# Products of zeros on TensorE in the waits of the first two units

## The reference

```python
for t in range(S):
    state = alpha[:, :, t, :, None] * state + np.einsum('bhd,bhe->bhde', k[:, :, t], v[:, :, t])
    y[:, :, t] = np.einsum('bhd,bhde->bhe', q[:, :, t], state)
```

## Time and profile before

| what | value |
|---|---|
| median of 3 runs | 1319.24 us |
| profiled execution | 1318.9 us |
| its span, first to last instruction | 1317.0 us |
| TensorE busy | 1300.2 us |
| mean granted TensorE clock | 0.997 |
| VectorE, ScalarE, GpSimd busy | 841.1, 607.8, 536.4 us |

### The profile page before, as it was taken

How to read it: one execution, slowest core, us unless ns; L and a number is a source line. 1 busy time by engine, 2 the same in 40 slices (tenths; PEclk the granted TensorE clock), 3 DMA queues, 4 the chain that set the end, 5 groups by cost and what they waited for, 6 DMA issues and landing times.

```text
span 1317.0 us, 26258 instructions
## 1 busy us (share of the span) xinstructions
PE 1300.2 (99%) x10472; PEld 1072.7 (81%) x10472; DVE 841.1 (64%) x1129; ACT 607.8 (46%) x1051; POOL 536.4 (41%) x454
## 2 busy tenths in 40 slices
PE   6999999999999999999999999999999999999999
PEld 6878888888888888888888888888888888888887
DVE  7787767665676765576766567676657645654455
ACT  3666343366434347533336743434753433653332
POOL 1671948611755831453861175583145311100011
PEclk9899999999999999999999999999999999999999
DMA  5535353255245236335335434423633332533330
GB/s 199 179 120 174 93 199 90 85 172 172 86 145 156 75 102 200 114 108 201 89 100 161 169 97 144 145 85 94 215 106 106 96 100 84 152 96 104 99 92 31
DMA packets 84028, 165.77 MB, mean 126 GB/s; under 512 B 30146, under 2 KB 31683, under 8 KB 83908
## 3 DMA queue, kind: packets, MB, share of 16 engines
q1 hardware_dynamic: 83616, 163.97, 39.9%
q10 hardware_dynamic: 292, 0.13, 0.0%
HBM read 157.99 MB, written 6.08 MB: 125 GB/s over the span
## 4 chain that ended last, share of the span: by engine, by line
PE 94%; DVE 3%; issue 1%; ACT 1%; DMA 0%; ACTq 0%; DVEq 0%
PE ps_o L578 15%; PE ps_h L578 14%; PE ps_h L579 14%; PE ps_h L580 14%; PE ps_o L579 14%; PE ps_o L580 14%; PE ps_att L450 2%; PE ps_att L547 1%; DVE w_lo L756 1%; PE ps_att L523 1%; PE ps_att L551 1%; PE ps_att L556 1%; PE ps_att L505 1%; DVE elu_out L769 1%; DVE g_lo L773 0%
## 5 line engine op out<-in xcount | busy, mean ns | idle before, releaser
L756 DVE TENSOR_TENSOR w_lo<-w_stage,w_hi 128x768 fp32r<-128x768 f32 x288 | 332.9, 1156 | 28.8 <-ACT w_hi L960 25.1
L578 PE MATMUL ps_o<-g_hi,w_lo 128*128 128x512 f32 x864 | 342.4, 396 | 0.3 <-DVE g_lo L773 0.3
L578 PE MATMUL ps_h<-x_hi,w_lo 128*128 128x512 f32 x858 | 335.1, 391 | 1.9 <-DVE x_lo L763 1.3
L579 PE MATMUL ps_o<-g_lo,w_hi 128*128 128x512 f32 x864 | 336.7, 390 | 0.0
L580 PE MATMUL ps_o<-g_hi,w_hi 128*128 128x512 f32 x864 | 336.6, 390 | 0.0
L579 PE MATMUL ps_h<-x_lo,w_hi 128*128 128x512 f32 x858 | 334.0, 389 | 0.0
L580 PE MATMUL ps_h<-x_hi,w_hi 128*128 128x512 f32 x858 | 333.9, 389 | 0.0
L991 ACT ACTIVATE g_hi<-ps_h 128x512 fp32r<-128x512 f32 x184 | 110.0, 598 | 473.9 <-PE ps_h L580 473.9
L777 DVE SCALAR_TENSOR_TENSOR g_lo<-ps_h,g_hi 128x512 fp32r<-128x512 f32 x184 | 126.9, 690 | 249.7 <-ACT g_hi L991 249.4
L960 ACT CAST w_hi<-w_stage 128x768 fp32r<-128x768 f32 x288 | 239.4, 832 | 13.9 <-DMA w_stage<-in_w 12.9
L285 POOL TENSOR_TENSOR products<-blocks 128x384 f32<-128x384 f32 x150 | 196.2, 1322 | 81.9 <-DVE scores L692 76.3
(11 more groups left out here) (111 smaller groups left out, 1025.5 us busy)
## 6 DMA issues: line engine op xcount, KB each, us to landing
w_stage<-in_w SPq DMA_DIRECT2D x288, 384.0 KB, 3.1
k_level<-in_k SPq DMA_DIRECT2D x12, 512.0 KB, 5.5
q_low<-in_q SPq DMA_DIRECT2D x12, 512.0 KB, 6.5
alpha<-in_a SPq DMA_DIRECT2D x12, 512.0 KB, 4.1
v_tok<-in_v SPq DMA_DIRECT2D x12, 512.0 KB, 4.7
p_rows<-p_norm SPq DMA_DIRECT2D x6, 1024.0 KB, 9.1
out<-acc SPq DMA_DIRECT2D x18, 256.0 KB, 4.3
blocks<-in_q_blocks SPq DMA_DIRECT2D x10, 384.0 KB, 4.0
```

The source lines that it names most:

```text
L578: nc.tensor.matmul(dst, lhs[1], rhs[0], start=first, stop=False)
L579: nc.tensor.matmul(dst, lhs[0], rhs[1], start=False, stop=False)
L756: nc.vector.tensor_tensor(wl[n % WRING][:], stage[n % STAGE][:], wh[n % WRING][:].bitcast(F32), ALU.subtract).then_inc(w_low, 1)
```

## The change

A helper `zeros(bank, count)` issues `count` products of a 128x128 stationary and a 128x128 moving operand, both the first 128 columns of the cleared buffer `SC[0]`. They write zeros into 128 columns of a bank that the next operation overwrites, and signal no semaphore. They are issued between two groups of waits, as follows: four ahead of the pairs (1, 4), two ahead of (1, 5), two ahead of (1, 6), four ahead of `transpose_k(0)`, three ahead of `outer(0)`: fifteen in all. In `early_pairs` the waits for `e_in`, `e_q` and `e_k` move behind those for `e_mask`, `e_rect` and `st_ready`, and behind the products of zeros; in `transpose_k` the two early waits change places. TensorE waits once for `sc_clear` behind the first state.

```diff
--- before.py
+++ after.py
@@ -105,6 +105,9 @@
 for lag in range(LEVELS - 2):
     EARLY_ORDER += [(0, lag + 2), (1, lag)]
 EARLY_ORDER += [(1, LEVELS - 2), (1, LEVELS - 1)]
+
+
+FILLED = {(1, LEVELS - 3): 4, (1, LEVELS - 2): 2, (1, LEVELS - 1): 2}
 
 
 
@@ -460,12 +463,12 @@
                     pe.wait_ge(k_up, lev(u, l - 1))
                 level(level_banks(u, l), u % 2, l).then_inc(step_done, 1)
 
+            def zeros(bank, count):
+
+                for i in range(count):
+                    nc.tensor.matmul(bank[:, 0:P], SC[0][:, 0:P], SC[0][:, 0:P], start=True, stop=True)
+
             def early_pairs(u, l):
-                if l == 0:
-                    pe.wait_ge(e_in[u], 32)
-                else:
-                    pe.wait_ge(e_q[u], l)
-                    pe.wait_ge(e_k[u], l)
                 if 2 <= l < MASKED + 2:
                     pe.wait_ge(e_mask[u], l - 1)
                 elif l >= MASKED + 2:
@@ -473,6 +476,12 @@
                 if u == 1 and l == 1:
                     pe.wait_ge(st_ready, 1)
                 banks = ps_l[l % 2][u]
+                zeros(banks[0], FILLED.get((u, l), 0))
+                if l == 0:
+                    pe.wait_ge(e_in[u], 32)
+                else:
+                    pe.wait_ge(e_q[u], l)
+                    pe.wait_ge(e_k[u], l)
                 if l == LEVELS - 1:
                     level(banks, u, l).then_inc(e_step[u], 1)
                     return
@@ -495,8 +504,9 @@
 
             def transpose_k(g):
                 if g < EARLY:
+                    pe.wait_ge(e_rect[g // 2], LEVELS - 1 - MASKED)
+                    zeros(kt_bank(g), 4 if g == 0 else 0)
                     pe.wait_ge(e_k[g // 2], LEVELS)
-                    pe.wait_ge(e_rect[g // 2], LEVELS - 1 - MASKED)
                 else:
                     pe.wait_ge(k_up, lev(g // 2, LEVELS - 1))
                     bank_free(g // 2, BANK_AT["K", 0] + g % 2)
@@ -509,6 +519,7 @@
             def outer(u):
                 if u < LEAD:
                     pe.wait_ge(e_rect[u], LEVELS - MASKED)
+                    zeros(kv_bank(u), 3 if u == 0 else 0)
                 else:
                     bank_free(u, BANK_AT["KV", 0])
                 o, s = kv_bank(u), u % 2
@@ -619,6 +630,7 @@
                 last.then_inc(o_step, 1)
 
             first_state()
+            pe.wait_ge(sc_clear, 1)
             for u, l in EARLY_ORDER[:-2]:
                 early_pairs(u, l)
             pe.wait_ge(eye_in, 16)
```

## The result

The changed kernel took 1325.66 us in the median of five executions (1322.26 to 1326.57), the kernel before 1319.08 beside it (1318.95 to 1319.44). The ratio is 1.0044, with a 95% interval of 1.0033 to 1.0055. I had forecast 1318.6, with 1317.6 to 1320.6 as the range, and a chance of 0.05 to anything above 1321.9.

What follows compares the result with a forecast made beforehand. TensorE was taken as the bound, its first main product moving the end. Saving 3.0 us of cold work and giving 2.2 back, with late start and VectorE, left minus 0.6: 1318.6 us from 1319.24, range 1317.6 to 1320.6.

Steps and rivals of the forecast that it cites:

- The first steps: From (1, 4) towards `attend(0)`: clock held at 1.00, products of zeros 0.26 us each, pairs (1, 5) ending 37.0 instead of 37.56.
- steps 7 and 8: `attend(0)` takes 1.55 instead of 2.06 us, transposes 2 and 3 start 0.57 earlier; that lead lasts to the first main product.
- that 0.57: Transposes 2 and 3 start 0.57 us earlier, at 41.65; kept, it puts the first main product at 49.7 instead of 50.28.
- the sign that the prediction named for an error in step 7: Transposes 2 and 3 starting directly behind `attend(0)`, instead of waiting for VectorE's late update until 41.65 us.
- The floor I derived from ScalarE: `outer(1)` needs `k_tokens(3)`, ending at about 44.0 us, so it ends at best at 44.45 instead of 45.67: gain at most 1.2.
- The premise that the clock is up from 31 us and falls at 34.2: TensorE in the kernel before: full speed from about 31 to 34.2 us, then half clock for 6.8 us until 41.0.
- the clock falls all the same: Clock at 0.50 when the transposes start at 34.3 us, `attend(0)` ending 2.0 us later, total 1321.2 us; chance 0.12.

Runs made afterwards that it cites:

- e7: Changed kernel, with unit 2's queries and the loads queued behind them waiting for all four `attend` of units 0 and 1 instead of two: 1323.86 us.
- e2_wide: Changed kernel with products of zeros of 256 moving columns instead of 128, half as many (2, 1, 1, 2, 2): 1319.88 us.
- e4_bare: Changed kernel without any products of zeros, only the reordered waits and the one for `sc_clear`: 1319.29 us.
- e3: Changed kernel with the same fifteen products shrunk to 32 weight columns and 16 moving ones: 1324.65 us.
- e5: Changed kernel with eleven tiny products (32 weight columns, 16 moving; counts 4, 2, 2, 3, 0) instead of fifteen full ones: 1321.65 us.
- e8: Kernel before the change, with unit 2's queries and the loads behind them waiting for all four `attend` of units 0 and 1: 1321.12 us.
- e1: The changed kernel run again without any edit: 1324.26 us.
- e6: Changed kernel with thirteen tiny products (32 weight columns, 16 moving; counts 4, 2, 2, 4, 1) instead of fifteen full ones: 1323.65 us.
- e9: Changed kernel with nineteen tiny products (32 weight columns, 16 moving; counts 4, 2, 2, 4, 7) instead of fifteen full ones: 1324.10 us.
- e10: Changed kernel with eleven of its fifteen full products (4, 2, 2, 3, 0): 1321.87 us.

## Why the prediction was wrong

The first steps held. Against the forecast (in brackets) the trace has a filler every 0.25 us (0.26), the transposes at 34.40 (34.3), the pairs (1, 5) at 35.81 to 36.95 (35.85 to 37.0), and a clock of 1.00 throughout. The pairs (1, 4) started at 32.34 us (32.2), so ScalarE slid by 0.4 us, not 0.2, which put `outer(0)` at 38.12 (37.85) and `attend(0)` at 40.20 (39.9):

```profile
33.54 1.06 ACT L941 COPY blocks<-ps_att 16x128 f32<-16x128 f32 x4 [1.07 <-PE ps_o L495]
...
43.36 1.08 ACT L957 COPY k_tok<-ps_o 128x512 f32<-128x512 f32 x2
```

Those are terms that were a little off. What failed is steps 7 and 8, "the rest runs at full clock in both kernels and keeps that 0.57". `attend(0)` took 2.09 us instead of 1.55, with 0.48 from start to start at border 1985; `outer(1)` 1.30 instead of 0.88, with 0.41 at border 2241; and the last `attend` took a silence of 1.95 at border 2497. Transposes 2 and 3 started at 42.29, directly behind `attend(0)`, which is the sign that the prediction named for an error in step 7. The forecast's 49.7 for the first dense product and the measured 52.76 differ by 3.06 us: about 0.65 had been lost by `outer(1)`, 0.3 of it ScalarE's slide; 0.42 were lost in `outer(1)`, and 2.0 from its end to that product. I priced an added instruction by its time on the array and forgot that it also takes a place in the instruction stream. No rival had it, and the bound of the range rested on the engines' waits alone. The signs stood in the trace of before: two silences ended by "issue" at 16 and 20 us, which the prediction passes over, and the instruction queue in the page's DMA section.

The floor I derived from ScalarE (1.2 us of gain) was not the tightest either. From border 2241 to the first record behind 2497 it took 5.3 to 6.5 us wherever TensorE arrived early, and 3.7 us without the loads (e7); from 1985 to 2241 it took 4.0 and 5.0 us in the two traces of the changed kernel. `outer` and `attend` need 3.4 us for 256 instructions at full clock (45.75 to 49.11). So between 41 and 51 us TensorE, once at full speed, runs ahead of its instructions. That is one likely reason why a held clock brought nothing: e2_wide, at full clock from 32.2 us, has its first dense product at 51.41 us, e4_bare, whose clock rises only at 41.8, at 51.34. The same traces show a second reason, the fillers' own place. Those ahead of (1, 4) held its pairs in e2_wide back to 32.87 us, and ScalarE's chain behind them started at 34.07, against 33.14 before the change (and 33.99 in e4_bare, whose pairs ran at half clock). `outer(1)` then began at 45.28 in e2_wide and at 45.57 in e4_bare, so the held clock was worth 0.3 us there; border 2241 then took 0.61 us from start to start, against 0.35. No run separates the two reasons. I found no kernel among these that beats the one before.

The premise that the clock is up from 31 us and falls at 34.2 came from one execution. In eight of the twelve traces it rises between 30.4 and 32.2 us, in e3 at 36.0, and in e4, e5 and e8 only at 40.3 to 42.0, without a fall before. Executions without a trace can't tell the two cases apart, because the time ahead of the first change counts as 1.00 in the mean: of 21 executions of the kernel before, the six with a mean of 0.997 have a median of 1319.07 us, the fourteen with 1.000, which may have held the clock or got it late, one of 1319.62.

My rival "the clock falls all the same" named the right sign and, at 1321.2, a wrong cause. The clock did fall, in e1, e3, e6, e9 and e10, but at 51 to 55 us, at the end of the silence or shortly behind it. The change's own trace, with 1.95 us, and e5's, with 1.24, have a silence at that border and no fall behind it; the five traces without a silence above 0.31 us there have no late fall at all. How much of the way from 1322.3 to 1326.6 us this explains stays open: none of the change's slowest executions left a trace. e3's does, at 1325.72 us, with 6.8 us at 0.50 and 2.6 us more than before from the first dense product on; but e9's, with the clock at 0.50 from 50.9 to 57.8 us, took no more than 1322.56.

Open too is what remains when that stall is small or lies behind the first dense product: 2.5 us in the median with eleven products, and 2.7 us between e7 and e8.

## What to carry to other kernels

Where TensorE issues many small products, count instructions as well as time: find the records behind which it falls silent for no other engine's sake, see whether their numbers share a remainder by 256, and ask which code an insertion pushes over a border. Eight wide fillers cost little where fifteen narrow ones cost 5 us or more, though they gained nothing either, and a border that can't be met in time is best placed in slow code, as the kernel before has it; whether a place inside a wait is as good wasn't tried. And before keeping a clock up, check that the work behind it could have used the speed.

## What the runs showed of the hardware

- The instructions of TensorE arrive in packets of 16 KB, each 0.9 to 1.4 us long in the first 57 us of these traces. Where it was waiting, TensorE went on about 1.15 to 1.6 us after the packet had landed. With the loads of unit 2 on the DMA engines (87 to 101% busy in the change's trace) the packet with the block behind border 2497 started 2.8 to 4.2 us behind border 2241, and 1.4 us when they were moved away (e7).
- In e1 the clock went to 0.50 at 55.4 us for 3.4 us, behind an idle stretch of 2.51 us and a wait for x of 1.27; in e3 at 53.0 for 6.8 us, 0.2 us after an idle stretch of 2.78 and still ahead of the wait for x. In the change's trace 1.68 us of idle time and the same wait left it at 1.00.
- A granted clock of 1.00 ahead of the first change in a trace tells nothing: in e4_bare the rows have 1.00 throughout, and the pairs (1, 5) at 36.2 us take 1.93 us all the same, the time at half clock.
- A float32 128x128 product takes 0.25 us at full clock: four of them from 33.40 to 34.40 us after the change.
